# Linear attention beside a gated layer on one core: each chunk's state update moved into the slot of its y

## What is computed

```
for t in range(S):
    state = f[t] * state + outer(k[t], v[t])       # one 48x48 state per batch and head
    y[t] = q[t] @ state
```

## Time and profile before

| | |
|---|---|
| median of 3 runs | 1424.93 us (1424.27 to 1424.94) |
| the profiled execution, its own time | 1423.43 us |
| its span | 1421.7 us |
| TensorE busy | 1392.5 us, 98% of the span |
| VectorE, ScalarE, GpSimd busy | 916.3, 569.0, 626.3 us |
| half 0 alone | 0 to 64.2 us |
| the seven pairs | 64.2 to 603.6 us |
| last gated layer and experts | 603.6 to 1421.7 us |

### The profile page before, as it was taken

One profiled execution on the slowest core, in us unless ns is written; L12 is line 12 of the kernel. 1 busy time (PEld: TensorE's weight loads), 2 busy tenths in 40 slices (PEclk: granted clock), 3 DMA queues, 4 the chain that ended last, 5 costly groups with the idle time before them and its releaser, 6 DMA issues.

```text
span 1421.7 us, 20981 instructions
## 1 busy us (share of the span) xinstructions
PE 1392.5 (98%) x8092; PEld 1316.1 (93%) x8092; DVE 916.3 (64%) x1376; ACT 569.0 (40%) x975; POOL 626.3 (44%) x719
## 2 busy tenths in 40 slices
PE   7899999999999999999999999999999999999999
PEld 6799999999999999998999999999999999999998
DVE  7785847566675757346666666666666666666666
ACT  5563534444444535245323332333333333343331
POOL 8776555555473747356412121212212354344430
PEclk9999999999999999999999999999999999999999
DMA  9535243342516051032010010101011111322111
GB/s 155 108 96 75 68 54 84 43 95 32 106 20 118 11 94 35 3 106 72 23 34 28 18 34 23 32 14 34 12 34 52 38 34 58 99 67 67 45 56 45
DMA packets 239796, 79.00 MB, mean 56 GB/s; under 512 B 188752, under 2 KB 238160, under 8 KB 239696
## 3 DMA queue, kind: packets, MB, share of 16 engines
q1 hardware_dynamic: 239696, 77.66, 24.0%
HBM read 67.83 MB, written 9.78 MB: 55 GB/s over the span
## 4 chain that ended last, share of the span: by engine, by line
PE 91%; POOL 2%; DVE 2%; ACT 2%; issue 1%; SPq 1%; DMA 1%; POOLq 0%; ACTq 0%; DVEq 0%
PE bank L1757 9%; PE bank L1755 9%; PE bank L1756 9%; PE bank L1705 8%; PE bank L1706 8%; PE bank L1704 8%; PE bank L1576 6%; PE bank L1668 4%; PE bank L1669 4%; PE bank L1670 4%; PE bank L1504 4%; PE bank L1503 4%; PE bank L1502 4%; PE bank L1608 3%; PE bank L1616 1%
## 5 line engine op out<-in xcount | busy, mean ns | idle before, releaser
L1458 DVE SCALAR_TENSOR_TENSOR acc<-bank,p_n,acc 128x384 f32<-128x384 f32 x384 | 234.7, 612 | 67.4 <-PE bank L1757 62.5
L788 POOL TENSOR_TENSOR g_l<-sig,g_h 128x384 fp32r<-128x384 f32 x128 | 161.2, 1260 | 238.0 <-ACT g_h L1026 238.0
L1757 PE MATMUL bank<-w_h,h_l 128*128 128x384 f32 x768 | 257.2, 335 | 0.0
L1755 PE MATMUL bank<-w_h,h_h 128*128 128x384 f32 x768 | 257.1, 335 | 0.0
L1756 PE MATMUL bank<-w_l,h_h 128*128 128x384 f32 x768 | 256.9, 334 | 0.0
L1442 DVE TENSOR_TENSOR bank<-bank,x_copy 128x512 f32<-128x512 f32 x192 | 124.6, 695 | 164.5 <-ACT x_copy L1126 101.9
L1704 PE MATMUL bank<-xs,we_h 128*128 128x512 f32 x528 | 205.5, 389 | 1.1 <-DVE h_l L1448 1.1
L1706 PE MATMUL bank<-xs,we_l 128*128 128x512 f32 x528 | 206.4, 391 | 0.0
L1705 PE MATMUL bank<-xs,we_h 128*128 128x512 f32 x528 | 206.3, 391 | 0.0
L839 POOL TENSOR_TENSOR we_l<-we_raw,we_h 128x384 fp32r<-128x384 f32 x96 | 96.8, 1033 | 217.1 <-ACT we_h L1092 217.1
L1354 DVE TENSOR_TENSOR sig<-bank,sig 128x384 f32<-128x384 f32 x128 | 71.0, 554 | 176.8 <-ACT sig L1019 175.4
(11 more groups left out here) (145 smaller groups left out, 2577.5 us busy)
## 6 DMA issues: line engine op xcount, KB each, us to landing
we_raw<-in_moe_w SPq DMA_DIRECT2D x32, 384.0 KB, 4.3
w_raw<-in_moe_w SPq DMA_DIRECT2D x32, 384.0 KB, 3.3
v_sb<-in_v SPq DMA_DIRECT2D x24, 192.0 KB, 3.6
x_dram<-work SPq DMA_DIRECT2D x8, 576.0 KB, 3.1
x_raw<-x_dram SPq DMA_DIRECT2D x12, 384.0 KB, 4.0
f_raw<-in_f_logit SPq DMA_DIRECT2D x56, 72.0 KB, 2.1
q_raw<-in_q SPq DMA_DIRECT2D x56, 72.0 KB, 2.1
k_raw<-in_k SPq DMA_DIRECT2D x56, 72.0 KB, 2.0
```

Of the source, the lines that this page charges most:

```text
L788: pool.tensor_tensor(g_l[:, j % RING, :], sig[:, j % 2, :], g_h[:, j % RING, :].bitcast(F32), ALU.subtract).then_inc(gl_ready, 1)
L1458: dve.scalar_tensor_tensor(acc[:, pr * TT + i, :], y_bank[y % 3][:, 0:DM], p_n[:, col:col + 1], acc[:, pr * TT + i, :], ALU.mult, ALU.add) ...
L1755: pe.matmul(dst, hh, wh, start=f == 0, stop=False)
L1757: last = pe.matmul(dst, hl, wh, start=False, stop=f == 1)
```

## The change

In `plan`, `update` of chunk c moves from the slot behind y (12, 14, 16) into the slot of y itself (11, 13, 15), right behind y. No instruction is added or removed, and no wait is.

```
--- before.py
+++ after.py
@@ -333,8 +333,8 @@
     plan[9] += [("k_rows", 0)]
     plan[10] += [("band", c) for c in range(CH)]
     for c in range(CH):
-        plan[11 + 2 * c] += [("y", c)]
-        plan[12 + 2 * c] += [("update", c)] + [("k_rows", c + 1)] * (c + 1 < CH) + [("x", c)]
+        plan[11 + 2 * c] += [("y", c), ("update", c)]
+        plan[12 + 2 * c] += [("k_rows", c + 1)] * (c + 1 < CH) + [("x", c)]
 
     plan[12] += [("next_sigmoid", 0)]
     plan[13].insert(0, ("next_turn", 0))
```

## The result

The changed kernel ran in 1416.51 us (median of 6, 1415.07 to 1417.31), the kernel before in 1424.93 (median of 6, 1424.2 to 1428.05): a ratio of 0.9936, with a 95% interval of 0.9926 to 0.9946. In two later comparisons, on two different chips, copies of the changed kernel gave 1416.57 and 1417.89, with ratios of 0.9951 and 0.9954 to the kernel before (6.8 and 5.8 us between the medians); the forecast's ratio, 0.9961, lies inside the intervals of these two (0.9935 to 0.9967, 0.994 to 0.9968) and outside that of the first. So the mechanism came as forecast, and what is to be explained is a part of 0.3 to 2.9 us that changes from one comparison to the next. Four runs of all that follow, of 1727, 2803, 3568 and 7915 us, are left out of every count of runs.

The account below looks back on a forecast made before the run. TensorE was taken as the bound: its products plus the places where it stands still. Gains of 5.3 us (y 1) and 0.2 (half 0), all else zero, made 5.5 off 1424.93: 1419.4 us, range 1417.8 to 1422.0.

Parts of the forecast that it names:

- The wait of y 1: In the pairs of halves 1 to 6, y 1 waits on TensorE for VectorE's state; removing this gains 5.3 us.
- The 0.11 for the held weight load: y 1's weight load on TensorE is held by the same wait, costing 0.11 us; otherwise the gain is 0.7 less.
- Rooms on VectorE and GpSimd: Instructions queued behind the moved state on VectorE, and g_l before layer_out 15, keep 4.6, 3.7 and 0.54 us room; cost zero.
- Rival C: GpSimd is held by the moved state in pairs of halves 2, 4, 6; g_l 15 late: 1430.4 us, chance 0.03.
- A: The wait comes again at layer_out 15, giving back 0.31 us a pair: 1421.3 us; chance 0.09.
- B: Another release as late stands behind the same wait, so y 1 still starts at 355.2: 1424.9 us, chance 0.07.
- Half 0, 0.2 us: In half 0 a GpSimd weight piece passes the last four decays; gain between 0 and 0.94 us, taken as 0.2.
- the sum: 5.3 us for y 1 in six pairs plus 0.2 in half 0: 5.5 us off the median, giving 1419.4.
- such a place: A place in TensorE's list of products where TensorE stands still; only these could be gained by reordering.
- The granted clock of 1.00: In the seven pairs TensorE's clock was read as 1.00, the higher of its two levels, 2.4 GHz.
- the difference of the profiled executions: The same 5.5 us was taken off the profiled execution, 1423.43 to 1417.9, and the median, 1424.93 to 1419.4.

Follow-up runs that it names:

- copy first: The kernel before, with GpSimd's g_l 9 made to wait for VectorE's first band copy: 1429.35 us, ratio 1.0022 to the kernel before.

## Why the prediction was wrong in size

The direction and the mechanism came as said; the size was 5.5 in place of 8.4 us.

*The wait of y 1, 5.3 us: right.* The table of the two profiles has 5.1 (0.82 to 0.91 in each pair; y 1 itself gains 0.85 or 0.91, and about 0.04 of that is paid back, since y's last products and the update's take 0.94 + 0.83 us from start to start behind each other, and took 0.87 + 0.86 in separate slots). Moving only update 0, or only the gates' sigmoid, removes the same waits; moving only updates 1 and 2 gives nothing.

*The 0.11 for the held weight load: right*, since 1.89 us per y came out whole; by the Trainium skill's rule that loads are pulled ahead of matmuls in flight (TensorE: Matmul & The Clock Gate, Architectural detail), taken to hold across a wait too, it would not have.

*Rooms on VectorE and GpSimd, costed at nothing: right.* 4.5 us where I gave about five, 0.54 at g_l 15. Rival C didn't come: g_l 15 took 1.01 and the decays 1.29. Neither did A or B.

*Half 0, 0.2 us: not supported.* The 0.25 between 76.8 us and y 0 of the first pair is in the change, but the unchanged copy of before has it too (0.26), so it is not the moved weight piece but what changes from run to run.

*The step that failed is the sum: it has no term for y 0.* The prediction says that "an edit that only reorders can gain nothing but such a place", and then lists such places from one profile and leaves y 0 out, at nothing and without a reason. Its 0.23 us of idle under the name "issue" stood beside the state in the list of waits, 0.4 us from start to start in six pairs. Under rival B the band copies are called "long done"; that holds for y 1, but the first copy ends 0.09 us before y 0 starts. The copy and g_l start within 20 ns of each other in six pairs, and which one is held changes from run to run. The first profile of before drew five losses of six, the first of after none: 1.6 to 2 us that no reading of the order could give, but that the range had to hold. That the median fell below the range in the first comparison may in part be such a draw; in the third, where the changed kernel's profile drew five losses, it was 1417.89, inside it.

Two more things were taken from a single profiled execution. The granted clock of 1.00 in the pairs was read as saying that the wait cost its length and nothing more. Behind the same 0.58 us of idle the clock fell in two profiles of near versions (updates 1 and 2 moved; copy first), at a cost of 1.65 and 1.6 us each. How often it does so in the kernel before no profile shows. And I set the difference of the profiled executions equal to that of the medians; they differed by 1.9 us, while the start of y 0 in the first pair alone moves by 1.3 us between profiles of the changed kernel.

Of the 8.4 us, then, 5.1 are shown as the wait, and about 1.7 as the race, in the one pair of profiles. The other 1.9 lie between those profiles and the medians, in runs that left no profile. More lost races, the clock behind the wait, a g_l of 4.65 us and the start of the first pair can each make such a difference; which of them did stays open. The third profile of the changed kernel, with five lost races and no waits of y 1, has 5.0 us less span than the first profile of before, which also lost five of the six: with the draw equal, the difference is near the 5.1 of the wait.

**Open.** Whether the change shifts the odds of the race. Late y 0, of six: 5, 4 and 5 where updates 1 and 2 stand at their old place and the copies in slot 10 (before twice, update 0 alone), and 5 with the sigmoid moved; 0, 3 and 5 for the whole change, 1 with updates 1 and 2 moved. That leans to one side, but four profiles on either side don't settle it, and no path from those updates to slot 10 is known. The clean control, the kernel before with its third copy behind the update, was not run.

## What to carry to other kernels

An instruction that nobody needs soon can hold one that somebody waits for: here the gates' sigmoid, two engines away, held up a PSUM bank. Look at what stands ahead of the late instruction on its own in-order engine, and move the one whose inputs have long been ready. An idle time of half a microsecond on TensorE cost 1.6 us more than its length in two places, because the clock fell behind it; such a wait can be worth removing beyond its price. The mean clock of a run doesn't say where it fell: look at it by stretches. And before a gain of a few microseconds is forecast, take every short idle of the bounding engine, the ones called "issue" too, and ask whether it is decided by two engines that start together; if it is, put it into the range, once for each pair.

## What the runs showed of the hardware

A COPY_PREDICATED of 1.36 us on VectorE and a TENSOR_TENSOR of 1.01 us on GpSimd that start within 20 ns of each other, GpSimd first, come out in three ways: 2.22 and 1.01, 1.36 and 2.20, or 1.36 for all three copies and 4.65. The same program shows all three, from one run to the next. The start alone doesn't decide who is held. In the first pair, where g_l starts 0.15 to 0.17 us ahead, it took 1.01 or 1.02 and the copy 2.05 to 2.10 in all eight profiles that leave this order alone. And g_l, made to start 1.43 us behind the first copy and so 0.2 us into the second, took 3.2 us in the other six pairs: it ended only after the third copy had.

The 4.65 us case in the profile after, pair of half 2:

```profile
188.65 4.64 POOL L788 TENSOR_TENSOR g_l<-sig,g_h 128x384 fp32r<-128x384 f32 x1 [1.71 <-ACT g_h L1026]
```

TensorE's clock can fall behind an idle time of 0.58 us: the granted clock was 0.70 and 0.75 over the five microseconds behind two such waits, and no such fall stands behind the twelve waits in the two profiles of the kernel before. Behind waits of 2.6 to 2.7 us, and one of 1.35, it fell in all seven pairs, and where it stood at 0.50 the products took twice as long. The Trainium skill (TensorE: Matmul & The Clock Gate, A second HAM failure mode: psum-queue depth-cycling) tells of a kernel whose matmul groups had small idle times between them, and whose clock went up and down. The trace agrees in part: the clock went from 1.00 to 0.70 and back behind one idle time of 0.58 us, but a single one, and only sometimes.
